# Normalising attention by scaling the probabilities ahead of their transposition instead of scaling a pair's outputs

## The reference, cut to what matters

```python
q_rot, k_rot = (rotate(q), rotate(k))                # 2 batches, 8 heads, 576 tokens, head_dim 64
scores = scale * np.matmul(q_rot, k_rot.transpose(0, 1, 3, 2))
scores = scores - np.max(scores, axis=-1, keepdims=True)
attn = np.exp(scores)
attn = attn / (np.sum(attn, axis=-1, keepdims=True) + 1e-09)
attn_out = np.matmul(attn, v)
x = attn_out                                         # as 1152 tokens x 512
h = x @ w_in; x = (h * sigmoid(h)) @ w_out           # 512 -> 2048 -> 512
h = x @ w_in2; return elu(h) @ w_out2                # 512 -> 2048 -> 512
```

## Time and profile before

| | |
|---|---|
| median of 3 runs | 562.24 us (561.94 to 562.62) |
| profiled execution | 561.98 us, of which the span is 560.2 us |
| TensorE matmul busy | 536.2 us, 96% of the span |
| VectorE busy | 279.0 us, 50% |
| ScalarE busy | 344.6 us, 62% |
| GpSimd busy | 347.5 us, 62% |
| granted TensorE clock | 1.000 |
| attention of chunk 0 alone | to about 64 us |
| units of chunk 0 with attention of chunk 1 | about 64 to 249 us |
| units of chunk 1 with attention of chunk 2 | about 249 to 424 us |
| units of chunk 2 alone | about 424 us to the end |

### The profile page before, as it was taken

The page is one execution under the profiler, slowest core; times in us unless marked ns, Lnnn a source line. Parts: engine busy times, 40 slices in busy tenths (PEclk is TensorE's granted clock), DMA queues, the critical chain, the costliest instruction groups (busy, mean ns, idle before and its releaser), DMA issues.

```text
span 560.2 us, 9272 instructions
## 1 busy us (share of the span) xinstructions
PE 536.2 (96%) x3308; PEld 529.0 (94%) x3308; DVE 279.0 (50%) x503; ACT 344.6 (62%) x726; POOL 347.5 (62%) x287
## 2 busy tenths in 40 slices
PE   1888889999999999999999999999999999999997
PEld 1777889999999999999999999999999999999997
DVE  5788755633258762336563237884334440057400
ACT  4899777755467765557775457775555663366531
POOL 6989989659646565645655654454544666656652
PEclk9999999999999999999999999999999999999999
DMA  8676735365254353344434442334333434334440
GB/s 332 199 219 187 204 102 179 103 198 160 95 166 138 99 165 124 113 116 152 124 108 142 117 117 91 116 105 136 111 108 110 131 129 134 123 124 131 130 144 29
DMA packets 43229, 77.16 MB, mean 138 GB/s; under 512 B 5296, under 2 KB 12848, under 8 KB 43184
## 3 DMA queue, kind: packets, MB, share of 16 engines
q1 hardware_dynamic: 41456, 74.21, 42.8%
q10 hardware_dynamic: 1728, 2.36, 1.1%
HBM read 63.57 MB, written 2.36 MB: 118 GB/s over the span
## 4 chain that ended last, share of the span: by engine, by line
PE 92%; ACT 3%; DVE 3%; issue 1%; DMA 1%; SPq 0%; ACTq 0%; DVEq 0%
PE banks L914 71%; PE banks L879 6%; PE banks L849 5%; PE banks L833 3%; PE banks L835 3%; PE banks L858 1%; ACT prob L449 1%; DVE neg_max L619 1%; PE banks L881 1%; DMA k_raw<-k 1%; PE banks L892 1%; DVE head_out L656 0%; ACT q_raw L434 0%; ACT k_st L419 0%; DVE pt_lo L626 0%
## 5 line engine op out<-in xcount | busy, mean ns | idle before, releaser
L331 POOL TENSOR_TENSOR w_lo<-w_raw,w_hi 128x512 fp32r<-128x512 f32 x192 | 246.8, 1288 | 194.8 <-ACT w_hi L489 194.5
L489 ACT CAST w_hi<-w_raw 128x512 fp32r<-128x512 f32 x189 | 117.7, 624 | 45.1 <-PE banks L914 41.2
L914 PE MATMUL banks<-x_lo,w_hi 128*128 128x384 f32 x384 | 129.8, 338 | 1.4 <-DVE x_lo L661 0.7
L914 PE MATMUL banks<-g_lo,w_hi 128*128 128x384 f32 x384 | 129.3, 337 | 0.0
L914 PE MATMUL banks<-g_hi,w_lo 128*128 128x384 f32 x384 | 128.7, 335 | 0.0
L914 PE MATMUL banks<-x_hi,w_lo 128*128 128x384 f32 x384 | 128.7, 335 | 0.0
L914 PE MATMUL banks<-x_hi,w_hi 128*128 128x384 f32 x384 | 128.5, 335 | 0.0
L914 PE MATMUL banks<-g_hi,w_hi 128*128 128x384 f32 x384 | 128.5, 335 | 0.0
L619 DVE TENSOR_REDUCE neg_max<-banks 128x1 f32<-128x576 f32 x72 | 54.3, 754 | 70.8 <-PE banks L835 69.4
L501 ACT ACTIVATE act_buf<-banks 128x384 f32<-128x384 f32 x96 | 47.2, 492 | 58.0 <-PE banks L914 57.7
L914 PEld LDWEIGHTS banks<-x_lo,w_hi 128*128 128x128 f32 x384 | 72.1, 188 | 3.1 <-DVE x_lo L661 1.6
(11 more groups left out here) (75 smaller groups left out, 723.2 us busy)
## 6 DMA issues: line engine op xcount, KB each, us to landing
w_raw<-w SPq DMA_DIRECT2D x192, 256.0 KB, 2.6
q_raw<-q SPq DMA_DIRECT2D x11, 384.0 KB, 3.1
q_one<-q_raw SPq DMA_DIRECT2D x44, 96.0 KB, 2.6
k_raw<-k SPq DMA_DIRECT2D x7, 576.0 KB, 4.6
k_st<-k_raw SPq DMA_DIRECT2D x28, 144.0 KB, 2.5
v_raw<-v SPq DMA_DIRECT2D x8, 320.0 KB, 3.0
out<-act_buf ACTq DMA_DIRECT2D x12, 192.0 KB, 2.5
q_two<-q_raw SPq DMA_DIRECT2D x22, 96.0 KB, 2.3
```

The costliest lines, as they stand in the source:

```text
L331: nc.gpsimd.tensor_tensor(w_st[LO][:, slot, :], w_raw[:, slot, :], w_st[HI][:, slot, :].bitcast(F32), ALU.subtract).then_inc(w_lo_done, 1)
L489: nc.scalar.copy(w_st[HI][:, slot, :], w_raw[:, slot, :]).then_inc(w_hi_done, 1)
L914: last = nc.tensor.matmul(dst, w_st[wp][:, slot, m * P:(m + 1) * P], src[xp][:, tile, :], start=start and n == 0, stop=stop and n == 2)
```

## The change

For tiles of chunk 0 (0 to 23) nothing changes. For tiles 24 to 71 VectorE, once the exponential is done, reduces the two slots of `row_sum`, takes the reciprocal and multiplies the 128 x 576 probabilities in place by it (`scale_tile`). It stands in VectorE's queue one unit after the one in which the tile's maximum was taken, behind `evict_first`, `evict_lo` and `evict_second`; tile 24 has it at unit 1. `transpose_tile` waits for `scaled` instead of `exp_done`. `invert_sums`, `widen_sums`, `spread_sums` and `scale_outputs` are gone for pairs 4 to 11; `output_hi` waits for the second head's `out_added` there. Three waits on `out_scaled` or `eps_done` go with them.

```diff
+            def scale_tile(n):
+                i, t, m = n // QN, n % QN, n - H * QN
+                dve.wait_ge(exp_done, n + 1)
+                nc.vector.tensor_reduce(tile_sum[:, :], row_sum[:, i // 2 % 2, t, i % 2, :], AXES.X, ALU.add) \
+                    .then_inc(sum_done, 1)
+                dve.wait_ge(sum_done, m + 1)
+                nc.vector.reciprocal(tile_inv[:, :], tile_sum[:, :]).then_inc(tile_inverted, 1)
+                dve.wait_ge(tile_inverted, m + 1)
+                nc.vector.tensor_scalar(prob[:, n % 3, :], prob[:, n % 3, :], tile_inv[:, 0:1], None, ALU.mult) \
+                    .then_inc(scaled, 1)
...
                 evict_lo(n - 2)
                 evict_second(n - 1)
+                if beside and j and tile_at(i, j - 1) is not None and QN * i + tile_at(i, j - 1) + 1 < STEPS:
+                    scale_tile(QN * i + tile_at(i, j - 1) + 1)
+                if n == 1:
+                    scale_tile(H * QN)
                 if i % H == 0 and i <= ITERS and j == 0:
                     if n == 0:
                         add_outputs(i - 1)
-                    scale_outputs(p - 1)
+                        scale_outputs(p - 1)
                     output_lo(p - 1)
...
-                if i % H == H - 1:
-                    if j == 6:
-                        invert_sums(p)
-                    if j == 7:
-                        add_outputs(i)
+                if i % H == H - 1 and j == 7:
+                    add_outputs(i)
                 if not first:
-                    if i % 2 == 0 and j == 1:
-                        invert_sums(p - 1)
                     if j == (3 if i % H == H - 1 else 4):
                         add_outputs(i - 1)
-                    if i % 2 == 0 and j == 6:
-                        scale_outputs(p - 1)
...
             def transpose_tile(n):
                 i, t = n // QN, n % QN
-                pe.wait_ge(exp_done, n + 1)
+                if n < H * QN:
+                    pe.wait_ge(exp_done, n + 1)
+                else:
+                    pe.wait_ge(scaled, n - H * QN + 1)
...
             def output_hi(p):
-                act.wait_ge(out_scaled, p + 1)
+                if p < 4:
+                    act.wait_ge(out_scaled, p + 1)
+                else:
+                    act.wait_ge(out_added, 2 * p + 2)
...
-                    hidden_unit(start, range(1))
-                    spread_sums(ahead // 2 - 1)
-                    hidden_unit(start, range(1, KT - 1))
+                    hidden_unit(start, range(KT - 1))
                     hidden_unit(start + 1, range(KT - 1))
...
-                        if j == 6 and i % 2 == 0 and u >= 8:
-                            spread_sums(i // 2 - 1)
```

More of the change, by code:

```diff
@@ L70, in build @@
         inv_wide = sb("inv_wide", [P, QN, 2, D])
+        tile_sum = sb("tile_sum", [P, 1])
+        tile_inv = sb("tile_inv", [P, 1])
         head_out = [sb(f"head_out{n}", [P, CT]) for n in range(2)]
@@ L90, in inv_rows @@
         def inv_rows(p):
-            return banks[:, 4 if p % 4 == 3 else PV_BANK, 0:CT]
+            return banks[:, 4 if p == 3 else PV_BANK, 0:CT]
         def scores(n):
@@ L167, in build @@
         eps_done, inv_done, inv_wide_done, row_done = sem("eps_done"), sem("inv_done"), sem("inv_wide_done"), sem("row_done")
+        sum_done, tile_inverted, scaled = sem("sum_done"), sem("tile_inverted"), sem("scaled")
         pv_done = sem("pv_done")
@@ L446, in exp_tile @@
                     act.wait_ge(end_transposed, n - 2)
-                if t == 0 and i % 2 == 0 and i >= 4:
+                if t == 0 and i % 2 == 0 and 4 <= i < 12:
                     act.wait_ge(eps_done, i // 2 - 1)
@@ L594, in _ @@
                 if j == 2 and not first:
-                    if i % 2 == 0:
-                        widen_sums(p - 1)
                     copy_out_lo(i - 1)
                 if i % H == H - 1 and j == 7:
-                    widen_sums(p)
                     copy_out_lo(i)
@@ L845, in transpose_tile @@
                     pe.wait_ge(pt_lo_done, n - 1 if n < H * QN else n)
-                if n in (H * QN, 2 * H * QN):
+                if n == H * QN:
                     pe.wait_ge(out_scaled, i // 2)
@@ L866, in value_products @@
                     pe.wait_ge(v_lo_done, i // 2 + 1)
-                if i % 2:
+                if i % 2 or i > H:
                     pe.wait_ge(out_added, i)
@@ L886, in spread_sums @@
                 pe.wait_ge(inv_wide_done, p + 1)
-                if p % 4 == 3:
+                if p == 3:
                     pe.wait_ge(pt_lo_done, QN * 2 * (p + 1))
```

## The result

The changed kernel takes 576.09 us (median of 6 runs, 574.15 to 576.77) against 562.43 us for the kernel before in the same comparison: a ratio of 1.0241, 95% interval 1.0229 to 1.0252. The forecast was 574.9 us, range 569.0 to 577.5. The profiled execution has 576.13 us, its span is 574.3 us: 14.1 us more than before, where 12.7 were forecast.

A forecast was written before the change was run, and what follows sets the result against it. TensorE, with 92% of the chain, was taken to bound the kernel, so its waits are lost in full. 14.7 us lost less 2.0 gained gave +12.7, 574.9 us on the median of 562.24; range 569.0 to 577.5.

The forecast's parts named there:

- the 13 places: Tile 24 and twelve tiles transposed at `j = 5`, where TensorE would wait for the scaling; 14.7 us lost in all.
- 35 tiles: The other tiles scaled, such as those transposed at `j = 3` or 0: scaling in time, nothing lost.
- The collision with GpSimd: The multiplication on VectorE waits for GpSimd's running instruction to end, then takes 0.42 us (bounds 0.19 to 0.62).
- The gain on TensorE: Eight spreads of sums go; six between output or hidden units save 0.33 us each, 2.0 us in all.
- the row behind `x_hi`: At the starts of chunks 1 and 2, `x_lo` ends as before, so the two spreads removed there gain nothing.
- tiles 24 and 25: First tiles scaled: tile 24 2.0 us late, net 1.05; tile 25 0.7 us, taken between 0 and 1.3.
- the two waits given up: TensorE's waits behind tile 24, 0.51 us at 75.92 and 0.43 by 78.43, expected to go once tile 24 is late.
- the other eleven late tiles: First layer: three hidden at 1.31 us, four outputs at 0.94; second layer: four hidden at 1.32; totals 3.9, 3.8, 5.3.
- (a): Rival: no collision, the multiplication takes 0.76 us whatever GpSimd does; +7.3 us, 569.5 us; chance 0.15.
- (b): Rival: no collision and half the streaming time, multiplication 0.45 us; +3.3 us, 565.5 us; chance 0.07.
- (c): Rival: 0.62 us behind GpSimd (2.6 more, 577.5 us), and VectorE falling behind in second layer's hidden units; chance 0.08.
- (d): Rival: not slower, TensorE's stalls are given back by later waits, leaving only the 2.0 us gain, 560.2 us; chance 0.03.

The follow-up runs named there:

- Experiment 8: Changed kernel with only scalings of tiles in a hurry moved ahead of `evict_first`, and tile 24's to the stage before: 559.55 us, 0.9946 of the kernel before.
- experiment 3: Changed kernel with the reciprocal written to a PSUM column and the multiplication a `tensor_tensor` with it: 570.35 us, 1.0146 of the kernel before.
- experiment 4: Changed kernel with the multiplication covering 8 of the 576 columns: 570.73 us, 1.0153 of the kernel before.
- 7: Changed kernel with GpSimd's weight subtraction covering 128 of 512 columns from unit 4 on: 566.79 us, 1.0081 of the kernel before.
- The removal alone: Changed kernel without the scaling at all, tiles 24 to 71 transposed when their exponential is done: 559.56 us, 0.9957 of the kernel before.
- experiment 10: Changed kernel with only tile 24's scaling issued and waited for, tiles 25 to 71 unnormalised: 561.73 us, 0.9981 of the kernel before.
- experiment 2: Changed kernel with the scaling (384 columns) written to a buffer nobody reads, transposition waiting for the exponential: 561.23 us, 0.9981 of the kernel before.

## Why the prediction was right

**The bound, and the places.** That any wait of TensorE's is lost in full, unless one behind it is given up, was right: the growth of each late tile stays to the end, but for tile 24. So were the 13 places, and that 35 tiles cost nothing; it followed from what stands ahead of the scaling in VectorE's queue. Experiment 8 shows it from the other side: the same 48 scalings cost 14.6 us of the stretch or nothing, by their place.

**The collision with GpSimd.** Taken from `x_lo`'s stretched instances; shown by experiments 3 (another operand, constant 0.75 us), 4 (eight columns, 0.92 us) and 7 (GpSimd out of the way, 0.52). What differed is the size behind the wait: 0.31 us where I took 0.42 from a row of another width and kind. That makes each lateness 0.1 us smaller than forecast, 1.31 to some 1.22. At tile 24 the 2.0 us came out by luck: two short instructions of GpSimd stood directly behind its subtraction, which ended at 75.57, and the multiplication ended at 76.17, 0.31 behind the second of them and 0.60 behind the subtraction.

```profile
74.61 1.56 DVE L667 TENSOR_SCALAR prob<-prob,tile_inv 128x576 f32<-128x576 f32 x1
75.50 0.20 POOL L389 MEMSET q_one<- 128x128 f32 x1
75.65 0.20 POOL L390 MEMSET q_two<- 128x128 f32 x1
```

The 0.52 us of an undisturbed multiplication shows why 0.42 was too large: at the 1.04 ns per element of the earlier trace rows it would be 0.75. By the Trainium skill (VectorE: DVE Perf Modes, "The perf-mode tier table") an fp32 `tensor_scalar` in SBUF runs at double rate, and my estimate from it, 0.32, agrees with the 0.31 of the trace. So does the Trainium skill's port rule (SBUF — State Buffer, "Who interferes with whom"), which names `tensor_scalar` in a two-port mode beside the instructions with two SBUF inputs: the rows of before showed only the latter, and this instruction has one and waits just the same, up to 1.56 us where it takes 0.52 alone.

**The gain on TensorE.** Forecast 2.0 us, 0.33 for each of six; measured 0.35 each, and about 0.05 at each chunk start, as the row behind `x_hi` had said. The removal alone gives 2.87; the other 0.7 was not in the sum and stays unexplained.

**What the sum lacked.** The clock. At tiles 24 and 25 I had 1.75 us in all, and 3.7 were measured. The difference of 2.0 has these parts: about 1.5 is the clock's; tile 25 is some 1.2 late from start to start instead of 0.7; tile 24 is 0.1 later; and the two waits given up gave back 1.1 instead of 0.95, since I had taken the first by its idle time (0.51), which is 0.15 less than from start to start. The same working gives 1.5 for the clock in experiment 10, where tile 25 doesn't wait. Against these 2.0 us more stand the other eleven late tiles, 0.9 us cheaper (12.1 against 13.0), and the gain, 0.9 larger. Then come some 0.05 us that show behind each late tile, while TensorE gets back into step, and that I had left out, 0.7 in all. That makes most of the 1.1 us between 13.8 and 12.7; the profiled execution grew by another 0.3, which lies ahead of tile 24, where two executions differ anyway. So the 574.9 came nearer to 576.09 than its terms deserve: errors of 1.8 us down and 2.7 up partly cancel. I had looked at the clock of the kernel before, 1.000 through all its waits, and concluded nothing from it; there the longest wait after the start is 1.4 us.

**Rivals.** (a) and (b) fall with the durations, as the change was made; (a) was built as experiment 3 and came 0.85 us above its number. (c): the part behind GpSimd's end is 0.31 and not 0.62, and VectorE falling behind is small, 1.5 us in experiment 2. (d), stalls given back, holds at tile 24 alone, and there for half of the wait.

## What to carry to other kernels

An instruction that another engine waits for is priced by its place in its own engine's queue first: find the last thing ahead of it that waits for the waiting engine itself. In this full pipeline the place alone was worth 14.6 us over 48 scalings, and only the instructions in a hurry should be moved up, since those moved without need delay the evictions behind them. Of an elementwise instruction that stays within SBUF ask what GpSimd does at that moment; with an operand in PSUM it can be slower alone and faster where it stands.

## What the runs showed of the hardware that was not expected

- A `tensor_scalar` of VectorE with one fp32 tensor input in SBUF and its output there waited for GpSimd's running SBUF instruction to end, however small it was itself: 128x8 took 0.92 us (0.23 alone), 128x576 1.21 (0.52 alone). It ended 0.31 us behind GpSimd's at 576 columns and 0.04 behind it at 8. A `tensor_tensor` with its second operand in PSUM took 0.75 us in 48 of 48 cases.
- After a wait of 2.0 us of TensorE, which came 9 products after one of 0.72, the granted clock was 0.5 (1.2 GHz) for some 3 us, and it cost 1.9 us, in 7 of 12 executions of one kernel and 5 of 6 of another. With a wait of 1.7 us at the same place (experiment 4) it stayed at 1.000 in four runs. What sets the limit between the two no run here shows.
